# Raw q and k transposed together, and split into parts afterwards by GpSimd

## The chip, the cores and the metric

The kernel runs on one core of a Trainium2 chip. A core has five engines that run their own instruction streams and meet at semaphores: TensorE (PE; its weight loads are listed apart, as PEld), VectorE (DVE), ScalarE (ACT), GpSimd (POOL) and SyncE (SP), from whose queue this kernel issues all its DMA transfers. The metric is device time in microseconds (us).

## What is computed

Attention with a bucket mask, and two feed-forward blocks behind it. For each of 2 x 8 heads (768 tokens, head dimension 64):

```python
q_bits = (einsum('bhsd,dk->bhsk', q, proj) > 0)      # proj: 64 x 6
k_bits = (einsum('bhsd,dk->bhsk', k, proj) > 0)
q_bucket, k_bucket = sum(q_bits * 2**arange(6)), sum(k_bits * 2**arange(6))
mask = q_bucket[..., :, None] == k_bucket[..., None, :]
scores = where(mask, q @ k.T / sqrt(64), -1e9)
attn = softmax(scores); o = attn @ v                 # [768, 64] per head
```

Then `h = (x @ w1) * (x @ w2)`, `x = h @ w3 @ w_out`, and four experts `relu(x @ w1[e]) @ w2[e]`, weighted and summed. All inputs and the output are float32.

## The kernel before

**Precision.** PE multiplies in the type fp32r. To keep float32 accuracy, every operand is split into a high part (`tensor_copy` into an fp32r tile) and a low part (the value minus its high part), and a product is the sum of high x high, high x low and low x high.

**Order of the work.** In the opening part (to about 66 us) `w3` is transposed and multiplied with `w_out`; the preparation of heads 0 and 1 is put between these matmuls (`first_prep(n)`, n from 0 to 13). Then comes attention, head by head: heads 0 and 1 unrolled, the next in a loop over pairs of heads, the last pair unrolled. Behind it come the gates (the two products with `moe_w1` and `moe_w2`), the product with w3 x w_out, and the experts. Each engine has an `attention(i, first, last)` in which the order of its work for one head, m = 2i + s, is written out by hand. "Stretch of a head" below means the time in which PE goes once through this order. For head m PE does:

score tiles 3 to 5 of head m, score tiles 0 to 2 of head m+1 (`scores`), six tiles of transposed exponentials (`transpose_exps`), the products with v (`multiply_pv`), and, spread over the stretch, the preparation of head m+2 (`prep`, `project_parts`) up to the first half of its one-hot codes; the second half comes at the start of the next stretch.

**Preparation of a head.** SP loads raw q and raw k (`load_qk`, 192 KB each, two heads ahead of their use). GpSimd splits each into high and low parts side by side, so that `q_parts` holds [q_hi | q_lo] and `k_parts` [k_lo | k_hi] for each of the six token tiles (`split_q`, `split_k`, lines 471 to 487). PE transposes the twelve tiles of 128 x 128 into one PSUM bank, `ps_prep`, three at a time: steps j = 0 to 3 of `prep` (L1373). ACT copies each three out (`prep_copy`, L720) into `q_cross` = [q_hi; q_lo] and `k_cross` = [k_lo; k_hi] (rows 0 to 63; rows 64 to 127). GpSimd stacks both high parts in `q_main` (`stack_highs`, L496). PE projects them (`project_parts`, L1390, and step j = 4, L1379), DVE turns the signs into `bits` (L996), PE multiplies these with the bucket codes in steps 5 and 6 (L1382), and DVE makes one-hot rows of them (`onehot`, L1000). SP moves the high part of k to rows 0 to 63 of `k_main` (`move_high`), and the one-hot rows into rows 64 to 127 of `q_main` and `k_main` (`move_onehots`), all from SBUF to SBUF (L328). A score tile is then q_main x k_main + q_cross x k_cross (L1410, L1412): the one-hot rows carry the mask.

**DVE and ACT in a stretch.** Per score tile DVE scales it and takes its extreme (`scale_scores`, L1006), ACT takes the exponential (`exp_tile`, L724). There is one score buffer (two PSUM banks), so `scores` waits until the tile before is scaled. Per tile of transposed exponentials ACT writes the high part (`pT_high`, L732) and DVE the low part (`pT_low`, L1024). ACT copies the lower half of a product with v (`o_lower`, L737, tile `o_low`), and DVE adds it to the upper half (`o_sum`, L1032). Once per head DVE adds 1e-9 to the six row sums (`guard_sums`, L1012: a tensor_scalar of 128 x 6 from SBUF to SBUF) and takes their reciprocals (L1018). The middle of DVE's order for a head reads:

```python
scale(1, 0); add_parts(-1, 1); guard_sums(m, s); pT_low(6*m + 3, 3)
scale(1, 1); reciprocals(m, ...); pT_low(6*m + 4, 4); scale(1, 2)
encode(2, 4); pT_low(6*m + 5, 5)
```

**GpSimd in a stretch.** `split_q`, `split_k` of head m+2, `split_v` of head m+1 (L506, L508), `stack_highs` of head m+2; in every second stretch `x_scale` (L517, two tensor_tensor on the output of the pair before), and from head 9 on `first_parts`, which prepares the gates' first operand (among it L558 and L560, a copy and a subtraction of 128 x 768). Behind attention GpSimd combines the first gate weights (L587 to L594) and splits them (L623, L625).

**SP in a stretch.** `move_onehots` (head m+1), `load_v`, `move_high` (head m+2), `load_qk` (head m+4), `spread_reciprocals` (row sums' reciprocals to DRAM, wait, and back, L319 and L323). These are in one queue, each with its waits.

Of the kernel before, what the change touches and what calls it, by code (L numbers as in the profile page):

```python
# [7 lines left out]
F32 = mybir.dt.float32  # L8
# [12 lines left out]
def build_program(nc, q, k, v, proj, moe_w1, moe_w2, moe_w3, moe_w_out, probs, moe2_w1, moe2_w2,  # L21
# [15 lines left out]
    GROUPS = 7  # L37
# [32 lines left out]
    with ExitStack() as ctx:  # L70
# [104 lines left out]
        raw_q = [place(f"raw_q{s}", [P, TILES, DH], F32, prep_at) for s in range(2)]  # L175
        raw_k = [place(f"raw_k{s}", [P, TILES, DH], F32, prep_at) for s in range(2)]
        q_parts = [place(f"q_parts{s}", [P, TILES, P], F32R, prep_at) for s in range(2)]
        k_parts = [place(f"k_parts{s}", [P, TILES, P], F32R, prep_at) for s in range(2)]
        proj_w = [place(f"proj_w{n}", [P, P], F32R, prep_at) for n in range(6)]
# [55 lines left out]
        v_loaded = [sem(f"v_loaded{n}") for n in range(2)]  # L235
        stacks_moved = [sem(f"stacks_moved{n}") for n in range(2)]
# [6 lines left out]
        gate_step, pool_held = sem("gate_step"), sem("pool_held")  # L243
# [3 lines left out]
        q_hi_done, k_hi_done, v_hi_done = sem("q_hi_done"), sem("k_hi_done"), sem("v_hi_done")  # L247
        q_split, k_split, v_split = sem("q_split"), sem("k_split"), sem("v_split")
        prep_mm, prep_copied, prep_coded = sem("prep_mm"), sem("prep_copied"), sem("prep_coded")
        prep_open, highs_stacked = sem("prep_open"), sem("highs_stacked")  # L250
# [31 lines left out]

        def up_step(e, h, j):
            return GATE_ALL + ROUND_STEPS * (ROUNDS * e + h) + j
# [13 lines left out]
        def _(sp):  # L298
# [27 lines left out]
            def move(s, *pairs):  # L326
                for dst, src in pairs:
                    sp.dma_start(dst.bitcast(F32), src.bitcast(F32)).then_inc(stacks_moved[s], 16)  # L328

            def move_high(m, s):  # L330

                sp.wait_ge(prep_copied, 4 * m + 4)
                move(s, (k_main[s][0:DH, :], k_cross[s][DH:P, :]))

            def move_onehots(m, s):

                sp.wait_ge(prep_coded, 3 * m + 3)
                move(s, (q_main[s][DH:P, :], onehot[0:DH, :]), (k_main[s][DH:P, :], onehot[DH:P, :]))
# [64 lines left out]
            def attention(i, first, last):  # L403

                for s in range(2):
                    if s or not first:
                        move_onehots(2 * i + s + 1, 1 - s)
                    load_v(i + 1, s, False)
                    move_high(2 * i + 2 + s, s)
                    if not last:  # L410
                        load_qk(i + 2, s, False)
                    spread_reciprocals(2 * i + s, i, s, first)

            for s in range(2):
                move_high(s, s)
                move_onehots(s, s)
# [11 lines left out]
            sp.wait_ge(q_split, HEADS)  # L428
# [37 lines left out]
        def _(pool):  # L466
# [4 lines left out]
            def split_q(m, i, s, first):  # L471

                if not first:
                    pool.wait_ge(prep_mm, GROUPS * (m - 2) + 4)
                pool.wait_ge(qk_loaded[s], 32 * (i + 1))
                held()
                nc.gpsimd.tensor_copy(q_parts[s][:, :, 0:DH], raw_q[s][:, :, :]).then_inc(q_hi_done, 1)
                pool.wait_ge(q_hi_done, m + 1)
                nc.gpsimd.tensor_tensor(q_parts[s][:, :, DH:P], raw_q[s][:, :, :],
                                        q_parts[s][:, :, 0:DH].bitcast(F32), ALU.subtract).then_inc(q_split, 1)  # L480

            def split_k(m, s):

                nc.gpsimd.tensor_copy(k_parts[s][:, :, DH:P], raw_k[s][:, :, :]).then_inc(k_hi_done, 1)
                pool.wait_ge(k_hi_done, m + 1)
                nc.gpsimd.tensor_tensor(k_parts[s][:, :, 0:DH], raw_k[s][:, :, :],
                                        k_parts[s][:, :, DH:P].bitcast(F32), ALU.subtract).then_inc(k_split, 1)

            def stack_highs(m, s, values):


                pool.wait_ge(v_split, values)
                for part, (rows, src) in enumerate(((slice(0, DH), q_cross), (slice(DH, P), k_cross))):
                    pool.wait_ge(prep_copied, 4 * m + 2 * part + 2)
                    held()
                    nc.gpsimd.tensor_copy(q_main[s][rows, :], src[s][rows, :].bitcast(F32)).then_inc(highs_stacked, 1)  # L496
                    pool.wait_ge(highs_stacked, 2 * m + part + 1)
                held()

# [20 lines left out]
            for n in range(6):  # L520
                nc.gpsimd.memset(proj_w[n][:, :].bitcast(F32), 0.0).then_inc(zeros_set, 1)
# [3 lines left out]
            for s in range(2):  # L525
                split_q(s, 0, s, True)
                split_k(s, s)
            split_v(0, 0, 0, True)
            for s in range(2):
                stack_highs(s, s, 1)  # L530
# [32 lines left out]
            def attention(i, first, last, parts=()):  # L563
                for s in range(2):
# [11 lines left out]
                    if not last:  # L576
                        stack_highs(m + 2, s, m + 2)
# [39 lines left out]

            pool.wait_ge(prep_mm, GROUPS * (HEADS - 1) + 4)
            pool.wait_ge(k_split, HEADS)
# [79 lines left out]
        def _(act):  # L699
# [15 lines left out]
            def prep_copy(m, s, j):  # L715

                act.wait_ge(prep_mm, GROUPS * m + j + 1)
                dst = (q_cross if j < 2 else k_cross)[s]
                half = slice((j % 2) * HALF, (j % 2 + 1) * HALF)
                nc.scalar.copy(dst[:, half], ps_prep[:, 0:HALF]).then_inc(prep_copied, 1)  # L720
# [24 lines left out]
            def attention(i, first, last):  # L745

                for s in range(2):
# [23 lines left out]
                    copy(2, 2)  # L771
# [4 lines left out]
                    copy(2, 3)  # L776
# [14 lines left out]
            def first_copy(n):  # L791
                if n % GROUPS < 4:
                    prep_copy(n // GROUPS, n // GROUPS, n % GROUPS)
# [176 lines left out]
        def _(dve):  # L970
# [20 lines left out]
            def prep_code(m, j):  # L991

                half = slice((j - 5) * HALF, (j - 4) * HALF)
                dve.wait_ge(prep_mm, GROUPS * m + j + 1)
                if j == 4:
# [46 lines left out]
            def attention(i, first, last):  # L1042

                for s in range(2):
# [14 lines left out]
                    encode(1, 5)  # L1059
                    scale(0, 3)  # L1060
                    add_parts(-1, 0)
                    encode(1, 6)
# [15 lines left out]
                    encode(2, 4)  # L1078
                    pT_low(6 * m + 5, 5)

            def constants():

                dve.wait_ge(const_loaded, 16 * (4 + B))
                dve.wait_ge(zeros_set, 7)
                nc.vector.tensor_copy(code[:, :, :], code_f[:, :, :]).then_inc(code_ready, 1)


                cols = [slice(c, c + BITS) for c in (0, KBIT, DH, DH + KBIT)]
                for n in range(4):
                    nc.vector.tensor_copy(proj_w[n + n // 2][:, cols[n]], proj_f[:, :]).then_inc(proj_hi_ready, 1)  # L1090
                dve.wait_ge(proj_hi_ready, 4)
                for n in range(4):
                    rows = slice(0, DH) if n % 2 == 0 else slice(DH, P)
                    nc.vector.tensor_tensor(proj_w[3 * (n // 2) + 2][rows, cols[n]], proj_f[rows, :],
                                            proj_w[n + n // 2][rows, cols[n]].bitcast(F32), ALU.subtract)\
                        .then_inc(proj_ready, 1)
# [10 lines left out]
            def first_code(n):  # L1107
                if n == GROUPS + 5:
                    dve.wait_ge(stacks_moved[0], 48)
                if n % GROUPS >= 4:  # L1110
                    prep_code(n // GROUPS, n % GROUPS)
# [209 lines left out]
        def _(pe):  # L1321
# [35 lines left out]
            def prep(m, s, j, first):  # L1357

# [3 lines left out]
                elif 1 <= j < 4:  # L1362
                    pe.wait_ge(prep_copied, 4 * m + j)
                elif j > 4:
                    pe.wait_ge(prep_coded, 3 * m + j - 4)
                if j == 0:
                    pe.wait_ge(q_split, m + 1)
                if j == 2:
                    pe.wait_ge(k_split, m + 1)
                if j < 4:  # L1370
                    parts = (q_parts if j < 2 else k_parts)[s]
                    for tt in range(HT):
                        last = nc.tensor.transpose(ps_prep[:, tt * P:(tt + 1) * P],  # L1373
                                                   parts[:, (j % 2) * HT + tt, :].bitcast(F32), ident[:, :])
                elif j == 4:

                    pe.wait_ge(highs_stacked, 2 * m + 2)
                    for h in range(2):
                        last = nc.tensor.matmul(ps_prep[:, 0:HALF], proj_w[3 * h + 2][:, :],  # L1379
                                                q_main[s][:, h * HALF:(h + 1) * HALF], start=False, stop=h == 1)  # L1380
                else:
                    last = nc.tensor.matmul(ps_prep[:, 0:HALF], code[:, j - 5, :], bits[:, :], start=True, stop=True)  # L1382
                last.then_inc(prep_mm, 1)

            def project_parts(m, s):

                pe.wait_ge(prep_copied, 4 * m + 4)
                for h in range(2):
                    for n, src in enumerate((q_cross, k_cross)):
                        nc.tensor.matmul(ps_prep[:, 0:HALF], proj_w[3 * h + n][:, :],  # L1390
# [318 lines left out]
```

## Time and profile before

| | |
|---|---|
| median of 3 runs | 992.93 us (992.86 to 993.02) |
| the profiled execution | 992.96 us |
| its span, first to last instruction | 991.2 us |
| PE busy | 984.3 us (99%) |
| DVE busy | 626.4 us (63%) |
| ACT busy | 464.3 us (47%) |
| GpSimd busy | 436.7 us (44%) |
| granted TensorE clock | 1.0 of full speed all through |
| attention, heads 0 to 15 | about 66 to 306 us |

Busy shares are averages over parts with different limits: DVE's 63% is 14.0 of 15.1 us in a head's stretch and far less in the experts. Rows below give times in us from the span's start; in a timeline a row is start, duration, engine, line, operation, tiles and shapes, and in square brackets the idle time of the engine ahead of it with what ended it.

### The profile page before, as it was taken

To read this page: it belongs to the slowest core of one execution; us is meant where nothing else is said; L and a number is where in the kernel's file an instruction comes from. 1 tells how busy PE (TensorE), PEld (TensorE's weight loads), DVE (VectorE), ACT (ScalarE), POOL (GpSimd) and SP (SyncE) were. 2 spreads that over 40 slices of the span, in tenths; PEclk is the share of its full clock that TensorE was granted. 3 is DMA by queue.
4 is the path that set the end of the run, shared out by engine and by line. 5 is a ranking of instruction groups with operands and counts; after the bars stand their busy time and mean duration, and the time that the engine had idled before them with its cause. 6 is when DMAs were issued, how large, how long until landed. Compare 5 with 4: busy or idle time off the path is not lost.

```text
span 991.2 us, 15991 instructions
## 1 busy us (share of the span) xinstructions
PE 984.3 (99%) x5494; PEld 917.4 (93%) x5494; DVE 626.4 (63%) x964; ACT 464.3 (47%) x853; POOL 436.7 (44%) x446
## 2 busy tenths in 40 slices
PE   9999999999999999999999999999999999999998
PEld 7889999999989999999998998989989899898997
DVE  6359999999997995598755352544535545355342
ACT  4248888888875543555542340422404224042230
POOL 4024445367797991694263160431604316043130
PEclk9999999999999999999999999999999999999999
DMA  6223333232233220101100111001110011010102
GB/s 245 88 65 89 90 103 87 80 107 86 70 84 93 64 64 22 43 22 43 44 22 22 55 31 43 22 22 50 37 36 29 21 45 40 31 32 21 43 22 105
DMA packets 57646, 57.44 MB, mean 58 GB/s; under 512 B 7552, under 2 KB 46592, under 8 KB 57600
## 3 DMA queue, kind: packets, MB, share of 16 engines
q1 hardware_dynamic: 57600, 56.85, 19.2%
q8 instruction: 26, 0.43, 0.2%
q14 instruction: 20, 0.16, 0.1%
HBM read 44.20 MB, written 3.19 MB: 48 GB/s over the span
## 4 chain that ended last, share of the span: by engine, by line
PE 98%; DVE 1%; ACT 0%; issue 0%
PE ps L291 24%; PE ps L292 24%; PE ps L293 24%; PE ps L1423 6%; PE ps L1410 3%; PE ps L1438 3%; PE ps L1412 3%; PE ps L1440 3%; PE ps L1373 2%; PE ps L1390 1%; PE ps L1332 1%; PE ps L1379 1%; PE ps L1325 1%; PE ps L1382 1%; DVE pT_lo L1024 0%; DVE expo L1006 0%
## 5 line engine op out<-in xcount | busy, mean ns | idle before, releaser
L636 POOL TENSOR_TENSOR v_sum<-kept,kept 128x384 f32<-128x384 f32 x48 | 51.8, 1080 | 287.3 <-ACT kept L822 287.3
L822 ACT COPY kept<-ps 128x384 f32<-128x384 f32 x144 | 67.7, 479 | 206.4 <-PE ps L293 205.4
L1300 DVE SCALAR_TENSOR_TENSOR acc<-ps,gate,acc 128x512 f32<-128x512 f32 x96 | 72.0, 750 | 139.5 <-PE ps L293 139.5
L293 PE MATMUL ps<-v_hi,hid_lo 128*128 128x512 f32 x384 | 149.6, 390 | 0.0
L292 PE MATMUL ps<-v_lo,hid_hi 128*128 128x512 f32 x384 | 149.5, 389 | 0.0
L291 PE MATMUL ps<-v_hi,hid_hi 128*128 128x512 f32 x384 | 149.4, 389 | 0.0
L1006 DVE TENSOR_SCALAR_CACHE_REDUCE expo<-ps 128x768 f32<-128x768 f32 x96 | 91.7, 956 | 14.2 <-PE ps L1412 10.6
L724 ACT ACTIVATE expo<-expo,neg_max 128x768 f32<-128x768 f32 x96 | 90.7, 945 | 5.9 <-DVE expo L1006 4.5
L1024 DVE TENSOR_TENSOR pT_lo<-ps,pT_hi 128x768 fp32r<-128x768 f32 x96 | 90.5, 947 | 1.6 <-ACT pT_hi L732 1.1
L1149 DVE TENSOR_TENSOR u_sum<-ps,kept 128x384 f32<-128x384 f32 x48 | 26.6, 554 | 100.5 <-PE ps L293 100.5
L732 ACT CAST pT_hi<-ps 128x768 fp32r<-128x768 f32 x96 | 76.9, 804 | 24.2 <-PE ps L1423 23.9
L293 PEld LDWEIGHTS ps<-v_hi,hid_lo 128*128 128x128 f32 x384 | 72.1, 188 | 14.9
L291 PEld LDWEIGHTS ps<-v_hi,hid_hi 128*128 128x128 f32 x384 | 72.1, 188 | 14.9
L292 PEld LDWEIGHTS ps<-v_lo,hid_hi 128*128 128x128 f32 x384 | 72.1, 188 | 14.8
L1287 DVE SCALAR_TENSOR_TENSOR hid_lo<-c,hid_hi 128x384 fp32r<-128x384 f32 x96 | 56.5, 601 | 36.5 <-ACT hid_hi L942 19.1
L1423 PE MATMUL ps<-ident,expo 128*128 128x128 f32 x576 | 75.7, 273 | 1.0 <-DVE pT_lo L1024 1.0
L291 PE MATMUL ps<-xc_hi,w_hi 128*128 128x384 f32 x224 | 75.8, 338 | 0.6 <-ACT kept L822 0.6
L292 PE MATMUL ps<-xc_lo,e_hi 128*128 128x384 f32 x224 | 75.7, 338 | 0.0
L293 PE MATMUL ps<-xc_hi,e_lo 128*128 128x384 f32 x224 | 75.7, 338 | 0.0
L293 PE MATMUL ps<-xc_hi,w_lo 128*128 128x384 f32 x224 | 75.7, 338 | 0.0
L292 PE MATMUL ps<-xc_lo,w_hi 128*128 128x384 f32 x224 | 75.7, 338 | 0.0
L291 PE MATMUL ps<-xc_hi,e_hi 128*128 128x384 f32 x224 | 75.7, 338 | 0.0
(164 smaller groups left out, 2529.6 us busy)
## 6 DMA issues: line engine op xcount, KB each, us to landing
w_raw<-in_moe_w SPq DMA_DIRECT2D x64, 128.0 KB, 2.4
e_raw<-in_moe_w SPq DMA_DIRECT2D x64, 128.0 KB, 2.4
v_raw<-in_moe_w SPq DMA_DIRECT2D x32, 256.0 KB, 3.1
w_raw<-in_moe_w SPq DMA_DIRECT2D x8, 512.0 KB, 3.7
raw_q<-in_q SPq DMA_DIRECT2D x16, 192.0 KB, 2.6
raw_k<-in_k SPq DMA_DIRECT2D x16, 192.0 KB, 2.6
raw_v<-in_v SPq DMA_DIRECT2D x16, 192.0 KB, 2.7
k_main<-k_cross SPq DMA_DIRECT2D x16, 192.0 KB, 2.7
```

Of the source, the lines that this page charges most:

```text
L291: nc.tensor.matmul(out_ps, lhs_hi, rhs_hi, start=start, stop=False, skip_group_check=onto)
L292: nc.tensor.matmul(out_ps, lhs_hi, rhs_lo, start=False, stop=False, skip_group_check=onto)
L293: return nc.tensor.matmul(out_ps, lhs_lo, rhs_hi, start=False, stop=stop, skip_group_check=onto)
L636: nc.gpsimd.tensor_tensor(v_sum[:, :], kept[s][1][:, :], kept[s][2][:, :], ALU.add).then_inc(v_done, 1)
L724: nc.scalar.activation(expo[slot][:, :], expo[slot][:, :], ACT.Exp, scale=-1.0, bias=neg_max[:, slot:slot + 1], accum_out=row_sum[s][:, t: ...
L732: nc.scalar.copy(dst, ps_pT[t % 2][:, :, 0:HALF].rearrange("p a (c n) -> p a c n", n=P))\
L822: nc.scalar.copy(kept[s][n][:, :], ps[4 * s + n][:, 0:HALF]).then_inc(kept_done, 1)
L1006: nc.vector.tensor_scalar(expo[slot][:, :].rearrange("p (a n) -> p a n", a=2), ps_score[:, :, 0:HALF], -SCALE, None, ALU.mult, ALU.min, ac ...
L1024: nc.vector.tensor_tensor(pT_lo[half][:, :, cols].rearrange("p (a c) n -> p a c n", a=2), ps_pT[t % 2][:, :, 0:HALF].rearrange("p a (c n) ...
L1287: nc.vector.scalar_tensor_tensor(hid_lo[:, tile, cols], src, 0.0, hid_hi[:, tile, cols].bitcast(F32), ALU.max, ALU.subtract).then_inc(hid_ ...
L1300: nc.vector.scalar_tensor_tensor(acc[:, t, :], ps[4 * ((h + t // 4) % 2) + t % 4], gate_f[:, bass.ds(t * E + e, 1)], acc[:, t, :], ALU.mul ...
L1423: last = nc.tensor.transpose(ps_pT[t % 2][:, kt // HT, (kt % HT) * P:(kt % HT + 1) * P], expo[slot][:, kt * P:(kt + 1) * P], ident[:, :])
```

## The change

Raw q and raw k of a head lie side by side in one tile, `raw_qk` ([128, 6 tiles, 2, 64], float32). PE transposes the six tiles of 128 x 128, three at a time, in steps 0 and 1; ACT copies each three into `qk_T`, of which rows 0 to 63 are q and rows 64 to 127 are k, still float32. When both halves are there, GpSimd copies the whole to `q_main` (high parts, [q_hi; k_hi]) and subtracts into `q_cross` (low parts, [q_lo; k_lo]): 128 x 768 each. The projection is rearranged to match, with as many matmuls as before: `project_highs` multiplies `q_main` with the high and low parts of `proj`, step 2 multiplies `q_cross` with the high ones. Steps 3 and 4 are the former 5 and 6. The parts are then brought to their rows by transfers: `move_k` (three: `k_main` and `k_cross` rows 0 to 63, `k_cross` rows 64 to 127) and `move_q` (one, `q_cross` rows 64 to 127, behind the projection and behind `move_k`'s landing), in place of `move_high`'s one. The loads of q and k write pieces of 64 floats, with a gap of 64 between them. PE's order in a stretch is the one before without the former steps 2 and 3; ACT's is without their copies.

```diff
             def load_qk(i, s, first):
                 if not first:
-                    sp.wait_ge(k_split, 2 * i + s - 1)
-                for raw, heads in ((raw_q, q_heads), (raw_k, k_heads)):
-                    sp.dma_start(raw[s][:, :, :].rearrange("p t d -> p (t d)"), heads[2 * i + s, :, :])\
+                    sp.wait_ge(prep_mm, GROUPS * (2 * i + s - 2) + 2)
+                for n, heads in enumerate((q_heads, k_heads)):
+                    sp.dma_start(raw_qk[s][:, :, n, :], heads[2 * i + s, :, :].rearrange("p (t d) -> p t d", d=DH))\
                         .then_inc(qk_loaded[s], 16)
...
-            def move_high(m, s):
-                sp.wait_ge(prep_copied, 4 * m + 4)
-                move(s, (k_main[s][0:DH, :], k_cross[s][DH:P, :]))
+            def move_k(m, s):
+                sp.wait_ge(qk_hi_done, m + 1)
+                move(parts_moved[s], (k_main[s][0:DH, :], q_main[s][DH:P, :]), (k_cross[s][0:DH, :], q_main[s][DH:P, :]))
+                sp.wait_ge(qk_split, m + 1)
+                move(parts_moved[s], (k_cross[s][DH:P, :], q_cross[s][DH:P, :]))
+
+            def move_q(m, i, s):
+                sp.wait_ge(parts_moved[s], 48 * (i + 1))
+                sp.sem_inc(sp_held, 1)
+                sp.wait_ge(prep_mm, GROUPS * m + 3)
+                move(stacks_moved[s], (q_cross[s][DH:P, :], q_main[s][0:DH, :]))
...
                     load_v(i + 1, s, False)
-                    move_high(2 * i + 2 + s, s)
+                    move_k(2 * i + 2 + s, s)
                     if not last:
                         load_qk(i + 2, s, False)
                     spread_reciprocals(2 * i + s, i, s, first)
+                    move_q(2 * i + 2 + s, i + 1, s)
...
+            def split_qk(m, s):
+                pool.wait_ge(prep_copied, 2 * m + 2)
                 held()
-                nc.gpsimd.tensor_copy(q_parts[s][:, :, 0:DH], raw_q[s][:, :, :]).then_inc(q_hi_done, 1)
...
+                nc.gpsimd.tensor_copy(q_main[s][:, :], qk_T[s][:, :]).then_inc(qk_hi_done, 1)
+                pool.wait_ge(qk_hi_done, m + 1)
+                held()
+                nc.gpsimd.tensor_tensor(q_cross[s][:, :], qk_T[s][:, :], q_main[s][:, :].bitcast(F32), ALU.subtract)\
+                    .then_inc(qk_split, 1)
...
                     if not last:
-                        split_q(m + 2, i + 1, s, False)
-                        split_k(m + 2, s)
+                        split_qk(m + 2, s)
...
-            def project_parts(m, s):
-                pe.wait_ge(prep_copied, 4 * m + 4)
+            def project_highs(m, s):
+                pe.wait_ge(prep_copied, 2 * m + 2)
+                pe.wait_ge(qk_hi_done, m + 1)
                 for h in range(2):
-                    for n, src in enumerate((q_cross, k_cross)):
...
+                    for n, w in enumerate((proj_hi, proj_lo)):
+                        nc.tensor.matmul(ps_prep[:, 0:HALF], w[h][:, :], q_main[s][:, h * HALF:(h + 1) * HALF],
+                                         start=h + n == 0, stop=False)
```

`held` is an increment of a semaphore that nobody waits for; it stands between two waits of an engine. In the opening part heads 0 and 1 keep their places in the order, with two of the seven places per head now empty, and GpSimd's first work is `split_v` of head 0.

## Rows read from the trace of the kernel before

**Rows 1.** The page: busy time of each engine.
```profile
PE 984.3 (99%) x5494; PEld 917.4 (93%) x5494; DVE 626.4 (63%) x964; ACT 464.3 (47%) x853; POOL 436.7 (44%) x446
```

**Rows 2.** Busy time by engine in one head's stretch of the steady loop.
```profile
186.40:201.50 15.10, 15.10 (x106) 14.69 (x105) 14.02 (x26) 13.01 (x26) 6.39 (x9) 1.00 0.33 91
```

**Rows 3.** The chain of waits: first three transpositions of two successive heads.
```profile
191.79 0.33 PE ps L1373 x3
...
206.86 0.33 PE ps L1373 x3
```

**Rows 4.** Timeline of DVE in that stretch: start, duration, work, idle before.
```profile
194.55 0.96 DVE L1006 TENSOR_SCALAR_CACHE_REDUCE expo<-ps 128x768 f32<-128x768 f32 x1
...
196.00 0.55 DVE L1032 TENSOR_TENSOR x_raw<-ps,o_low 64x384 f32 x1 [0.49 <-ACT o_low L737]
...
196.58 0.17 DVE L1012 TENSOR_SCALAR guarded<-row_sum 128x6 f32<-128x6 f32 x1
...
196.72 0.96 DVE L1024 TENSOR_TENSOR pT_lo<-ps,pT_hi 128x768 fp32r<-128x768 f32 x1
...
197.60 0.95 DVE L1006 TENSOR_SCALAR_CACHE_REDUCE expo<-ps 128x768 f32<-128x768 f32 x1
```

**Rows 5.** Timeline of PE and its weight loads in that stretch.
```profile
193.65 0.34 PE L1410 MATMUL ps<-k_main,q_main 128*128 128x384 f32 x1
...
198.65 0.42 PE L1410 MATMUL ps<-k_main,q_main 128*128 128x384 f32 x1
...
201.18 0.10 PEld L1382 LDWEIGHTS ps<-bits,code 128*128 128x128 bf16 x1 [0.16 <-DVE bits L996]
```

**Rows 6.** Timeline of ACT in that stretch.
```profile
193.50 0.48 ACT L720 CAST q_cross<-ps 128x384 fp32r<-128x384 f32 x1
...
194.87 0.49 ACT L720 CAST k_cross<-ps 128x384 fp32r<-128x384 f32 x1
...
195.38 0.48 ACT L737 COPY o_low<-ps 64x384 f32<-64x384 f32 x1
...
196.58 0.49 ACT L720 CAST k_cross<-ps 128x384 fp32r<-128x384 f32 x1
```

**Rows 7.** POOL: starts behind its waits (timeline), then groups by line and form.
```profile
197.22 0.83 POOL L496 CAST q_main<-k_cross 64x768 fp32r<-64x768 f32 x1 [0.64 <-ACT k_cross L720]
...
290.50 0.74 POOL L594 TENSOR_TENSOR w_raw<-w_raw 128x256 f32<-128x256 f32 x1 [0.18 <-POOL w_raw L591]
...
L560 POOL TENSOR_TENSOR xc_lo<-s_raw,xc_hi 128x768 fp32r<-128x768 f32 x4 | 7.4, 1850 | 0.3
```

**Rows 8.** Line L1012's durations (min/median/max), then timelines of DVE and POOL.
```profile
L1012 DVE TENSOR_SCALAR guarded<-row_sum x16: 153/172/705, 76.1 to 300.0; 128x6 f32<-128x6 f32 x16
...
285.88 2.35 POOL L517 TENSOR_TENSOR x_raw<-x_raw,rec_rows 128x384 f32<-128x384 f32 x2
...
286.40 0.70 DVE L1012 TENSOR_SCALAR guarded<-row_sum 128x6 f32<-128x6 f32 x1
...
298.55 1.83 POOL L625 TENSOR_TENSOR w_lo<-w_raw,w_hi 128x768 fp32r<-128x768 f32 x1
...
299.99 0.42 DVE L1012 TENSOR_SCALAR guarded<-row_sum 128x6 f32<-128x6 f32 x1
```

**Rows 9.** Timelines of POOL and PE where attention hands over to the gates.
```profile
273.54 0.83 POOL L558 CAST xc_hi<-s_raw 128x768 fp32r<-128x768 f32 x1 [0.17 <-POOL q_main L496]
...
297.80 0.42 PE L291 MATMUL ps<-xc_hi,w_hi 128*128 128x384 f32 x1
```

**Rows 10.** The page's DMA issues (median us to landing), SP's timeline, then tile k_main.
```profile
e_raw<-in_moe_w SPq DMA_DIRECT2D x64, 128.0 KB, 2.4
...
190.36 0.59 SPq L328 DMA_DIRECT2D k_main<-onehot  x1
...
201.19 0.54 SPq L323 DMA_DIRECT2D rec_rows<-sum_reciprocals  x1
...
DMA to landing us min/median/max: 2.5/2.9/4.5
```

More of the change, by code:

```diff
@@ L173, in build_program @@
         assert rec_at[0] <= cursor[0]
[L175 to L179, printed above, removed]
+        raw_qk = [place(f"raw_qk{s}", [P, TILES, 2, DH], F32, prep_at) for s in range(2)]
+        qk_T = [place(f"qk_T{s}", [P, S], F32, prep_at) for s in range(2)]
+        proj_hi = [place(f"proj_hi{h}", [P, P], F32R, prep_at) for h in range(2)]
+        proj_lo = [place(f"proj_lo{h}", [P, P], F32R, prep_at) for h in range(2)]
         onehot = place("onehot", [P, S], F32R, prep_at)
@@ L235, in build_program @@
         v_loaded = [sem(f"v_loaded{n}") for n in range(2)]
+        parts_moved = [sem(f"parts_moved{n}") for n in range(2)]
         stacks_moved = [sem(f"stacks_moved{n}") for n in range(2)]
@@ L412, in attention @@
                     spread_reciprocals(2 * i + s, i, s, first)
+                    move_q(2 * i + 2 + s, i + 1, s)
             for s in range(2):
-                move_high(s, s)
+                move_k(s, s)
+                move_q(s, 0, s)
                 move_onehots(s, s)
@@ L519, in _ @@
             nc.gpsimd.memset(ident[:, :], 0.0).then_inc(zeros_set, 1)
-            for n in range(6):
-                nc.gpsimd.memset(proj_w[n][:, :].bitcast(F32), 0.0).then_inc(zeros_set, 1)
+            for part in (*proj_hi, *proj_lo):
+                nc.gpsimd.memset(part[:, :].bitcast(F32), 0.0).then_inc(zeros_set, 1)
             pool.wait_ge(zeros_set, 1)
@@ L524, in _ @@
                                     pattern=[[-1, P]], channel_multiplier=1).then_inc(ident_ready, 1)
[L525 to L527 removed]
             split_v(0, 0, 0, True)
             for s in range(2):
[L530 removed]
+                split_qk(s, s)
             def first_parts(step):
@@ L717, in prep_copy @@
                 act.wait_ge(prep_mm, GROUPS * m + j + 1)
-                dst = (q_cross if j < 2 else k_cross)[s]
-                half = slice((j % 2) * HALF, (j % 2 + 1) * HALF)
-                nc.scalar.copy(dst[:, half], ps_prep[:, 0:HALF]).then_inc(prep_copied, 1)
+                nc.scalar.copy(qk_T[s][:, j * HALF:(j + 1) * HALF], ps_prep[:, 0:HALF]).then_inc(prep_copied, 1)
             def exp_tile(g, slot, s, t):
@@ L1366, in prep @@
                 if j == 0:
[L1367 to L1371, printed above, removed]
+                    pe.wait_ge(qk_loaded[s], 32 * (i + 1))
+                if j < 2:
                     for tt in range(HT):
[L1373 to L1377, printed above, removed]
+                        last = nc.tensor.transpose(ps_prep[:, tt * P:(tt + 1) * P], raw_qk[s][:, j * HT + tt, :, :].rearrange("p n d -> p (n d)"),
+                                                   ident[:, :])
+                elif j == 2:
+                    pe.wait_ge(qk_split, m + 1)
@@ L1378, in prep @@
                     for h in range(2):
-                        last = nc.tensor.matmul(ps_prep[:, 0:HALF], proj_w[3 * h + 2][:, :],
-                                                q_main[s][:, h * HALF:(h + 1) * HALF], start=False, stop=h == 1)
+                        last = nc.tensor.matmul(ps_prep[:, 0:HALF], proj_hi[h][:, :],
+                                                q_cross[s][:, h * HALF:(h + 1) * HALF], start=False, stop=h == 1)
                 else:
-                    last = nc.tensor.matmul(ps_prep[:, 0:HALF], code[:, j - 5, :], bits[:, :], start=True, stop=True)
+                    last = nc.tensor.matmul(ps_prep[:, 0:HALF], code[:, j - 3, :], bits[:, :], start=True, stop=True)
```

113 lines of the change are left out of this document (43 added, 70 removed).

## The prediction

> **What bounds the kernel now.** I read the page first: PE is busy for 984.3 us, 99% of the span [rows 1], so PE work that goes should be time that goes. Then I went to the stretches that the change touches, since a share over the span hides other limits there. While one head is attended, the stretch holds 15.10 us of PE work and, beside it, 14.02 us of DVE work [rows 2]. One head follows the other after 206.86 - 191.79 = 15.07 us [rows 3]. PE is the bound, with DVE only 1.1 us behind it, so the question is how the two engines are coupled.
>
> The timelines answer that for the second half of a head, in which all of the change's transpositions lie. DVE scales a score tile (L1006, 194.55), idles 0.49 us until ACT has copied `o_low`, adds (196.00), guards the row sums (L1012, 196.58), forms `pT_lo` (196.72) and scales the next tile (197.60 to 198.55) [rows 4]. `scores` waits for that scaling, since there is one score buffer, and PE's next score matmul starts at 198.65 [rows 5]: no slack. At 201.18 PE waits again, 0.16 us, for DVE's `bits` [rows 5]. So in this half of the head PE runs in DVE's step, and PE work taken out there is worth only what DVE gets earlier.
>
> **The change, part by part.** All times are of the stretch above; it stands for the 14 heads' stretches in which a head two ahead is prepared.
>
> PE: six of twelve transpositions per head go. Three take 0.33 us of the chain [rows 3], one 0.11. In the loop, 84 of them leave PE 0.66 us per head free. In the opening part, heads 0 and 1 are prepared between matmuls of the weight product, with nothing near them that PE waits for: 12 x 0.11 = 1.3 us gained there. The four matmuls of `project_highs` and the two of step 2 cost what `project_parts` and step 4 did.
>
> ACT: the two `k_cross` copies go. The first (194.87 to 195.36) stood right ahead of the `o_low` copy (195.38) [rows 6], which moves up by 0.49 us. That is DVE's idle time: its addition could then start when the scaling ends, at 195.54 in place of 196.00, and the guard at 196.12. PE meets the next scores 0.66 us earlier, so it isn't late for DVE's scaling. With nothing else in the way a head would take 0.46 us less.
>
> GpSimd: per head four splits and two stacking copies go; one copy 128x768 and one subtraction 128x768 come. The row of the copy says 0.83 us [rows 9], that of the same subtraction 1.85 us [rows 7]. Both wait for the second transposed half, whose copy ends at 193.50 + 0.48 = 193.98 [rows 6]. GpSimd started 0.15 us behind the ACT copy that ended at 196.58 + 0.49 = 197.07 [rows 6], at 197.22, and 0.18 us behind its own result when a wait and a `held` lie between [rows 7]. So: copy 194.13 to 194.96, subtraction 195.14 to 196.99. PE wants the copy in `project_highs`, which stands behind scores that wait for the scaling's end at 195.54: hidden by 0.6 us at least. It wants the subtraction behind the scores of 198.65: hidden by 1.7 us. Were that cover gone, each us late would be a us per head.
>
> But the guard would now start at 196.12, inside that subtraction. L1012 takes 0.15 to 0.25 us in fourteen heads, and 0.70 and 0.42 in two [rows 8]. In those two GpSimd was in a tensor_tensor: two of them from 285.88, the first over at about 285.88 + 2.35/2 = 287.06, the guard at 287.10; one over at 298.55 + 1.83 = 300.38, the guard at 300.41 [rows 8]. The guard ends 0.03 us behind the GpSimd instruction that it met, wherever in it it came. The `pT_lo` and PSUM-reading instructions show nothing of the sort: L1024 keeps to 0.96 us [rows 4]. So the new guard should last from 196.12 to 197.02, and `pT_lo` starts at about 196.94, against 196.72 before. DVE comes out 0.22 us later, not 0.46 earlier; with up to 0.06 us of slack at the score wait I take 0.21. Scores, scaling, `bits` and the code matmul behind them follow, each coupled as above, and the next head starts 0.21 us later: 14 x 0.21 = +2.9 us. Bounds per head: -0.46 (the guard isn't held) and +0.30 (subtraction late by a tenth).
>
> The Trainium skill, Advanced Engine Details and Errata, section VectorE Performance Modes, says that an instruction of VectorE that uses two ports (source and destination in SBUF) and GpSimd's instructions block each other, as the second port is shared. The guard is the one such instruction in the loop, and the two long guards agree; by a reading in which only GpSimd gives way, the sum would be that of the rival "the guard is free".
>
> GpSimd at the end of attention: its first copy of the parts that follow head 15's preparation starts at 273.54, and from there to PE's first gate matmul at 297.80 GpSimd is busy without a gap; PE gets there just as its operand is ready [rows 9]. The new order ends the preparation later: counted from 186.5, the subtraction is over at 10.5, and `split_v` (a copy and a subtraction of half the width, so a bit over half their 2.86 us, an estimate) and the starts behind it take until 12.25. In head 13's stretch, which begins five periods later at 261.85, that copy came at 11.7. It comes 0.55 later, of which PE itself loses 0.2: +0.35 us once.
>
> SP: three more transfers per head, each of the form of `k_main<-k_cross`. `move_k` ends its waits with the subtraction at 196.99, where `move_high` waited until 197.07; queued behind it are `load_qk` and the reciprocals, which nobody needs soon. `move_q` waits last, behind the reciprocals' round trip, whose last transfer was issued at 201.19 for 0.54 us [rows 10] and now comes 0.2 later: `move_q` has issued by about 202.4, one period earlier 187.3. `move_onehots` is next behind it, its two transfers issued about half a us apart, the second at 190.36 [rows 10]: 2.5 us to spare. The second lands 2.9 us later, 193.26 [rows 10], against scores that run at 193.65 [rows 5] with weights loaded 0.17 earlier: about 0.2 us of slack, unchanged, price 0. `load_qk` now writes 256 B pieces in place of 1,536 B ones. Loads in 512 B pieces land in 2.4 us (128 KB), moves in 3,072 B pieces in 2.9 (192 KB) [rows 10]: small pieces don't show in the landing. I take 0, since the loads have a whole head of time; the upper bound is a rival.
>
> Sum: -1.3 + 2.9 + 0.35 = +2.0 us. The profiled execution took 992.96 us (span 991.2 and 1.8 around it), the runs' median 992.93, so nothing is to be corrected: 994.9 us.
>
> **The rivals.**
>
> The guard is free. For it: two rows are few, and neither has a GpSimd subtraction from this very tile. Against it: both ends agree to 0.03 us. Then each of 14 heads gains 0.46 us, the opening 1.3, and the hand-over to the gates costs 1.0 (GpSimd 0.55 late, PE 0.46 early): 992.96 - 6.4 - 1.3 + 1.0 = 986.3.
>
> All PE time counts. For it: 99% [rows 1]. Against it: DVE's coupling at 198.65 and 201.18 [rows 5]. It gives 96 x 0.11 = 10.5 us, 982.5.
>
> The loads in small pieces hold up the queue. Raw loads stand ahead of the reciprocals' round trip, `move_q` and the onehots. Up to 2.7 us (2.5 + 0.2) of longer loads per head are free; from there PE waits at the first score of each head. At 4 us it would lose 1.3 us, and 14 heads 18 us, with the forecast's other terms 1013. Against it: the small pieces above.
>
> The Trainium skill, DMA: Bandwidth & Descriptors, section Specifications, gives 512 B as the least piece for full rate, with a read-modify-write below it. That speaks for this rival; no transfer of 256 B pieces is in this trace.
>
> **How the numbers follow.** The guard held: 0.65, own range 992.4 to 996.8 (low: 0.05 per head, 1.3 off, no hand-over; high: 0.30 per head, 1.0 off, hand-over 0.6). The guard free: 0.18. All PE time: 0.05. The queue held up: 0.12. About 0.2% (2.0 us) is what a measurement of this kernel can tell from no change: below 991.0 is faster, above 994.9 slower. The forecast lies on that edge, so its 0.65 goes to 0.31 slower, 0.32 same, 0.02 faster. Faster 0.25, same 0.32, slower 0.43. The range takes in the free guard, 985.2 to 998.0, and leaves out all PE time and most of the held queue.
>
> **What would show it.** L1012 at 0.8 to 0.95 us in the heads' stretches, ending with GpSimd's new subtraction; heads 15.2 to 15.35 us apart; no wait of PE for GpSimd in the loop; the opening 1.3 us shorter. Wrong would be: L1012 near 0.17 and heads 14.6 us apart; a wait of PE for an onehot transfer; a subtraction well off 1.85 us.

## The result, and the profile of the changed kernel

The changed kernel takes 996.42 us (median of 7 runs, 995.64 to 997.81), the kernel before 993.02 (7 runs, 992.58 to 994.25): ratio 1.0036 [1.0025 to 1.0048], slower by 0.36%. The forecast was 994.9 us, its range 985.2 to 998.0. The profiled execution took 995.64 us, its span is 993.8 against 991.2, +2.6.

The page of the changed kernel, first busy time by engine, then the DMA queue (packets, MB, share of 16 engines):
```profile
PE 978.9 (99%) x5398; PEld 905.3 (91%) x5398; DVE 633.6 (64%) x964; ACT 451.8 (45%) x821; POOL 403.5 (41%) x380
...
q1 hardware_dynamic: 81920, 66.29, 24.2%
```
Against [rows 1] PE lost 96 instructions and 5.4 us of busy time, ACT 12.5 us, GpSimd 33.2 us. DVE has the instructions that it had, 964, and 7.2 us more busy time. No work was given to it, so some instruction of it got longer. Which one shows in the groups for lines L997 (the guard, L1012 before), L1003 (the reciprocal) and L494 (GpSimd's new subtraction), in ns min/median/max:
```profile
L997 DVE TENSOR_SCALAR guarded<-row_sum x16: 424/947/1382, 74.4 to 302.4; 128x6 f32<-128x6 f32 x16
...
L1003 DVE RECIPROCAL row_rec<-guarded x16: 179/180/183, 77.0 to 304.0; 128x6 f32<-128x6 f32 x16
...
L494 POOL TENSOR_TENSOR q_cross<-qk_T,q_main x16: 1832/1842/1852, 23.4 to 272.7; 128x768 fp32r<-128x768 f32 x16
```
The same 128 x 6 instruction took a median of 172 ns before [rows 8] and takes 947 now.

Timeline of the stretch that answers to the one of [rows 3] to [rows 7], all engines, in order of time. First transpositions stand at 192.69 and 207.97: 15.28 us apart.
```profile
192.69 0.49 PE L1353 MATMUL ps<-ident,raw_qk 128*128 128x128 f32 x3
...
194.57 0.48 ACT L707 COPY qk_T<-ps 128x384 f32<-128x384 f32 x1
195.22 0.83 POOL L491 CAST q_main<-qk_T 128x768 fp32r<-128x768 f32 x1 [10.89 <-ACT qk_T L707]
...
195.62 0.96 DVE L991 TENSOR_SCALAR_CACHE_REDUCE expo<-ps 128x768 f32<-128x768 f32 x1
...
196.23 1.84 POOL L494 TENSOR_TENSOR q_cross<-qk_T,q_main 128x768 fp32r<-128x768 f32 x1 [0.18 <-POOL q_main L491]
...
196.62 0.55 DVE L1017 TENSOR_TENSOR x_raw<-ps,o_low 64x384 f32 x1
...
197.21 0.89 DVE L997 TENSOR_SCALAR guarded<-row_sum 128x6 f32<-128x6 f32 x1
198.01 0.94 DVE L1009 TENSOR_TENSOR pT_lo<-ps,pT_hi 128x768 fp32r<-128x768 f32 x1
...
199.10 0.85 PE L1405 MATMUL ps<-ident,expo 128*128 128x128 f32 x6 [0.44 <-DVE pT_lo L1009]
...
207.97 0.49 PE L1353 MATMUL ps<-ident,raw_qk 128*128 128x128 f32 x3
```
The reader is to see three things. The idle time ahead of DVE's addition (0.49 us in [rows 4]) is gone: it follows the scaling at once. The guard then starts 0.98 us into the subtraction, which ends at 196.23 + 1.84 = 198.07, and ends itself at 198.10. And PE, which stood still for nobody there before, waits 0.44 us for the `pT_lo` behind the guard. The table of the stretch (busy time of PE, PEld, DVE, ACT, POOL) and the waits of the whole span say the same, 7.1 us in 13 places:
```profile
192.69:207.97 15.28, 14.84 (x100) 14.03 (x98) 14.53 (x25) 12.19 (x24) 6.47 (x6) 1.00 0.53 132
...
PE ps L1405 <- DVE pT_lo L1009: 7.1, 13, 1.0
```
PE is busy for 0.23 us less in this window than the 15.07 of before, and the window is 0.21 us longer.

**Where the time went, on the trace.** The first transposition of head 2 moved from 71.29 to 69.97 (-1.32, the opening). The 13 periods from there to the last prepared head add up to 199.17 us against 195.66 (+3.51). From there to the first gate product, 300.26 against 297.80 [rows 9], another 0.27 was lost, and the rest, between 0.1 and 0.2, behind it: +2.6 together.

### The profile page after: what moved, and what is told of

It is laid out like the page before. It is cut to its first block, busy times and chain, and to the rows that moved or that the text cites. A ratio compares the mean times of both kernels' runs of the same rounds, so it can differ in the third digit from the quotient of the medians.

```text
span 993.8 us, 15662 instructions
## 1 busy us (share of the span) xinstructions
PE 978.9 (99%) x5398; PEld 905.3 (91%) x5398; DVE 633.6 (64%) x964; ACT 451.8 (45%) x821; POOL 403.5 (41%) x380
## 4 chain that ended last, share of the span: by engine, by line
PE 63%; POOL 1%; issue 0%; ACT 0%; DVE 0%; POOLq 0%; ACTq 0%
PE ps L295 21%; PE ps L296 21%; PE ps L297 21%; POOL w_raw L578 0%; POOL c L646 0%; POOL w_raw L582 0%; POOL a L631 0%; ACT w_hi L730 0%; POOL c L631 0%; POOL v_sum L625 0%; ACT kept L807 0%; POOL w_raw L585 0%; DVE acc L1283 0%; POOLq L484 0%; POOL w_raw L579 0%
## 5 line engine op out<-in xcount | busy, mean ns | idle before, releaser
L991 DVE TENSOR_SCALAR_CACHE_REDUCE expo<-ps 128x768 f32<-128x768 f32 x96 | 91.7, 955 | 14.6 <-PE ps L1394 11.1
L1009 DVE TENSOR_TENSOR pT_lo<-ps,pT_hi 128x768 fp32r<-128x768 f32 x96 | 90.3, 945 | 1.2 <-ACT pT_hi L719 1.2
L491 POOL CAST q_main<-qk_T 128x768 fp32r<-128x768 f32 x16 | 13.2, 824 | 162.8 <-ACT qk_T L707 162.8
L1405 PEld LDWEIGHTS ps<-ident,expo 128*128 128x128 f32 x576 | 65.7, 140 | 14.3 <-ACT expo L711 11.7
```

Source lines behind the costliest of these rows:

```text
L991: nc.vector.tensor_scalar(expo[slot][:, :].rearrange("p (a n) -> p a n", a=2), ps_score[:, :, 0:HALF], -SCALE, None, ALU.mult, ALU.min, ac ...
L1009: nc.vector.tensor_tensor(pT_lo[half][:, :, cols].rearrange("p (a c) n -> p a c n", a=2), ps_pT[t % 2][:, :, 0:HALF].rearrange("p a (c n) ...
L1405: last = nc.tensor.transpose(ps_pT[t % 2][:, kt // HT, (kt % HT) * P:(kt % HT + 1) * P], expo[slot][:, kt * P:(kt + 1) * P], ident[:, :])
```

## Experiments

A period is the time from one head's first transposition to the next's. Ratios are to the kernel before, measured in the same session. All edits are to the changed kernel unless said otherwise.

**1. No guard.** The addition of 1e-9 is left out and the reciprocal reads the row sums themselves.
```diff
-                nc.vector.tensor_scalar(guarded[:, :], row_sum[s][:, :], EPS, None, ALU.add).then_inc(sums_guarded, 1)
+                dve.sem_inc(sums_guarded, 1)
...
-                nc.vector.reciprocal(row_rec[:, :], guarded[:, :]).then_inc(rec_done, 1)
+                nc.vector.reciprocal(row_rec[:, :], row_sum[s][:, :]).then_inc(rec_done, 1)
```


> The changed kernel with the guard of the row sums left out: the reciprocals are taken of the row sums as they are (what is left out is the addition of 1e-9). If DVE's wait for GpSimd's subtraction is what turned the change into a loss: DVE gets its 0.46 us back and the guard's own 0.1, heads go from 15.28 to 14.5 us apart, and the whole to 986.5 us (14 heads x 0.76 and the odd starts of the subtraction off, the hand-over to the gates 0.8 on). If the loss comes from the transfers, the small load pieces or GpSimd's own lateness: heads stay near 15.3 us apart and the whole at 995 to 997.

988.72 us, ratio 0.9958 [0.9941 to 0.9975]: from slower to faster by one instruction of six columns. Ten of the 13 periods are 14.46 to 14.63 us, three 14.92 to 15.04. GpSimd's subtraction is as long as ever, and `pT_lo` (L1009) starts inside it:
```profile
189.89 0.96 DVE L991 TENSOR_SCALAR_CACHE_REDUCE expo<-ps 128x768 f32<-128x768 f32 x1
190.42 1.84 POOL L494 TENSOR_TENSOR q_cross<-qk_T,q_main 128x768 fp32r<-128x768 f32 x1 [0.18 <-POOL q_main L491]
...
191.53 0.96 DVE L1009 TENSOR_TENSOR pT_lo<-ps,pT_hi 128x768 fp32r<-128x768 f32 x1
...
291.52 0.41 PE L295 MATMUL ps<-xc_hi,w_hi 128*128 128x384 f32 x1 [1.24 <-issue]
```
`pT_lo` starts 1.64 us behind the scaling, where it was 2.39 in the changed kernel. The last row is the first gate product: with the heads shorter, PE gets there 1.24 us before its operand. In each of the three long periods PE waits for a transfer of one-hot rows (0.20, 0.23 and 0.34 us), of which experiment 5 shows more. The expectation was missed by 2.2 us: the periods are 14.6 and not 14.5, three of them are longer, and behind the first gate product this execution takes 2.1 us more than the changed kernel's, in waits among the gates (below). PE's wait ahead of that product was priced at 0.8.

**2. The kernel before without its guard**, as the control: the same edit to it.

> The kernel before with the guard left out (what is left out is the addition of 1e-9), the control for e1. There the guard takes 0.17 us and the tile that follows it waits for ACT until 0.14 us behind the guard's start, so nothing should be gained per head: 991.5 to 993 us, with about 0.7 us to be had only in the last two heads, where it met GpSimd. If leaving the guard out is worth as much here as in e1, the wait for GpSimd is not the change's own cost.

993.14 us, ratio 0.9999 [0.9990 to 1.0009]; periods 15.07. The guard's own 0.17 us is worth nothing. So experiment 1 is not the price of an instruction but of its wait. First gate product:
```profile
295.61 2.38 POOL L625 TENSOR_TENSOR w_lo<-w_raw,w_hi 128x1024 fp32r<-128x1024 f32 x1
...
298.09 0.42 PE L291 MATMUL ps<-xc_hi,w_hi 128*128 128x384 f32 x1 [0.74 <-issue]
```
In the last heads, where the guard took 0.70 and 0.42 [rows 8], PE came free sooner, and then waited 0.74 us. The profile names no releaser for that wait, but the product starts 0.10 us behind the end of GpSimd's first low part of the gate weights (295.61 + 2.38 = 297.99), and so it does in all twelve profiles. The hand-over to the gates goes by GpSimd.

**3. The subtraction in two halves** of 128 x 384.
```diff
-                nc.gpsimd.tensor_tensor(q_cross[s][:, :], qk_T[s][:, :], q_main[s][:, :].bitcast(F32), ALU.subtract)\
+                nc.gpsimd.tensor_tensor(q_cross[s][:, t0], qk_T[s][:, t0], q_main[s][:, t0].bitcast(F32), ALU.subtract)\
+                    .then_inc(half_split, 1)
+                nc.gpsimd.tensor_tensor(q_cross[s][:, t1], qk_T[s][:, t1], q_main[s][:, t1].bitcast(F32), ALU.subtract)\
```


> The changed kernel with GpSimd's subtraction 128x768 made as two of 128x384. If the guard waits for the end of the one GpSimd instruction that it meets: the first half should be over at about the time at which the guard starts, so L997 falls from 0.95 to 0.1 to 0.3 us, heads come to 14.6 to 14.7 us apart, the whole to about 988 us. If the guard has to wait until GpSimd is idle: no change or slower by the extra instruction, 996 to 998.

992.81 us (10 runs), ratio 0.9994 [0.9984 to 1.0004]: no change that could be measured, and 5 us more than expected. The periods alternate between about 14.63 and 15.40. Two neighbouring stretches, GpSimd's halves (L495, L497) and the guard (L1000):
```profile
178.52 1.01 POOL L495 TENSOR_TENSOR q_cross<-qk_T,q_main 128x384 fp32r<-128x384 f32 x1 [0.19 <-POOL q_main L492]
179.38 0.18 DVE L1000 TENSOR_SCALAR guarded<-row_sum 128x6 f32<-128x6 f32 x1
179.49 1.02 POOL L497 TENSOR_TENSOR q_cross<-qk_T,q_main 128x384 fp32r<-128x384 f32 x1
...
193.14 1.00 POOL L495 TENSOR_TENSOR q_cross<-qk_T,q_main 128x384 fp32r<-128x384 f32 x1 [0.18 <-POOL q_main L492]
194.11 1.01 POOL L497 TENSOR_TENSOR q_cross<-qk_T,q_main 128x384 fp32r<-128x384 f32 x1
194.12 1.03 DVE L1000 TENSOR_SCALAR guarded<-row_sum 128x6 f32<-128x6 f32 x1
```
A guard that is there 0.11 us before the second half starts slips in at the seam and costs 0.18; one that comes 0.01 behind its start waits it out, 194.11 + 1.01 = 195.12 against 195.15. The length of the wait is the rest of the one instruction met. My expectation had the guard meet the first half always; where in GpSimd's work it falls was known only to a tenth, and that tenth decided. The tenth is in the kernel before too: the guard starts 0.58 us behind the start of DVE's addition in one head and 0.47 in the next, in turn, in every profile with a guard on DVE. The 0.58 are the heads in which that addition writes rows 64 to 127, and the guard then starts behind the addition's end instead of 0.08 us ahead of it; why is not shown.

**4. The guard as a tensor_tensor**, which adds a tile that holds 1e-9: the same work on two operands in SBUF.
```diff
-                nc.vector.tensor_scalar(guarded[:, :], row_sum[s][:, :], EPS, None, ALU.add).then_inc(sums_guarded, 1)
+                nc.vector.tensor_tensor(guarded[:, :], row_sum[s][:, :], eps_t[:, :], ALU.add).then_inc(sums_guarded, 1)
```


> The changed kernel with the guard as a tensor_tensor with a tile of 1e-9 (two SBUF inputs) in place of a tensor_scalar. If only the two-port form of a one-input instruction is held: the guard takes about 0.2 us and the whole comes to 987. If anything that reads through DVE's second SBUF port is held, two inputs too: no change, 995 to 997, guard near 0.95 us.

996.48 us, ratio 1.0042 [1.0026 to 1.0059]. It is held just as long:
```profile
L999 DVE TENSOR_TENSOR guarded<-row_sum,eps_t x16: 429/942/1359, 74.2 to 302.7; 128x6 f32<-128x6 f32 x16
```

**5. The guard on ACT.** The whole computation stands; ACT adds 1e-9, behind `pT_high` of tile 4.
```diff
+            def guard_sums(m, s):
+                if not isinstance(m, int) or m:
+                    act.wait_ge(rec_done, m)
+                act.wait_ge(exp_done, 6 * m + TILES)
+                nc.scalar.activation(guarded[:, :], row_sum[s][:, :], ACT.Copy, bias=EPS).then_inc(sums_guarded, 1)
...
                     pT_high(6 * m + 4, 4)
+                    guard_sums(m, s)
```


> The changed kernel with the whole computation kept and the guard moved to ACT, behind the fifth tile of transposed exponentials (pT_high 4), where ACT has idle time. If DVE's wait for GpSimd is the cost: as e1, about 987 us; ACT's 0.2 us per head are hidden. If ACT has become too tight: 988 to 991.

989.90 us, ratio 0.9971 [0.9959 to 0.9984]. The guard takes 216 to 242 ns on ACT. Most of the other periods are 14.6, but six of 13 are 14.86 to 15.49. What PE waits for in them, in this kernel's waits (us in total, times, longest):
```profile
PE ps L1398 <- DMA k_main<-onehot: 2.5, 6, 0.7
...
PEld ps L1398 <- DMA k_main<-onehot: 1.3, 2, 0.9
```
The one-hot rows come too late in all six. (The two rows count one of these waits twice, and one of PEld's, 0.40 us in the last heads, is in the kernel before too, with 0.38.) So the rival of the held-up queue shows once the heads are quicker. At 15.28 us it hardly does: the changed kernel's profile has no such wait in the 13 periods, the second profile of it (experiment 10) one of 0.39 us that lengthens no period, and experiment 4's one of 0.58 us, in a period of 15.70.

**6. The guard on ACT, and `move_q` issued earlier**: between the store of the reciprocals and the wait for it, where the queue stood idle.
```diff
                 sp.dma_start(sum_rec_tiles[m, :, :], row_rec[:, :]).then_inc(rec_stored, 16)
+                if between is not None:
+                    between()
                 sp.wait_ge(rec_stored, 16 * (m + 1))
...
-                    spread_reciprocals(2 * i + s, i, s, first)
-                    move_q(2 * i + 2 + s, i + 1, s)
+                    spread_reciprocals(2 * i + s, i, s, first, lambda: move_q(2 * i + 2 + s, i + 1, s))
```


> e5 with one more edit on SP's queue: move_q is issued between the reciprocals' store and the wait for it, in place of behind their read-back. In e5 PE waited 3.8 us in eight heads for an onehot transfer. If those land late because move_q's transfer and the read-back are issued right ahead of them: the waits fall under 1 us, all heads come to 14.6 us apart, the whole to 986 to 987 us. If they are late for DMA traffic in general: as e5, 990.

987.12 us, ratio 0.9944 [0.9929 to 0.9959]. Behind the first, all periods are 14.61 to 14.68: no long one is left. PE still waits 1.20 us at the first gate product.

**7. The same, with GpSimd's preparation of the gates a step earlier.**
```diff
-            attention(DK + 2, False, False, ((3,), (4, 5)))
-            attention(PAIRS - 1, False, True, (6, 7))
+            attention(DK + 2, False, False, ((3, 4), (5, 6)))
+            attention(PAIRS - 1, False, True, (7,))
```


> e8 with GpSimd's first_parts moved up: step 4 from head 13's stretch to head 12's, steps 5 and 6 in head 13's, only step 7 in head 14's. In e1 and e5 PE waited 1.2 us at the first gate product for GpSimd's split weights. If GpSimd's unbroken work there is what PE meets: the wait goes and the whole is 1.0 to 1.2 us below e8, about 985.5. If the weights' loads end last: as e8.

986.00 us (5 runs, 985.39 to 988.59), ratio 0.9941 [0.9927 to 0.9954]. First gate product:
```profile
290.51 0.42 PE L295 MATMUL ps<-xc_hi,w_hi 128*128 128x384 f32 x1 [0.24 <-issue]
```
It starts 1.44 us earlier than in experiment 6 (0.34 of that stands already in its opening), and the span is 1.4 shorter (984.1 against 985.5), though the intervals of the two ratios overlap. This version computes all that the reference does and is faster than both kernels: 0.6% less than the one before, and by the two ratios about 1% less than the changed one.

**8. The changed kernel with `move_q` earlier and nothing else.**

> The changed kernel with only SP's order changed as in e8. If the guard's wait sets the pace of the heads, the transfers do not: 995.5 to 997, as the changed kernel, perhaps with fewer slow runs. If late onehot transfers made the part of the loss that the profile of the fastest run does not show: 995 and a spread under 1 us.

996.84 us, ratio 1.0040 [1.0024 to 1.0055]: nothing gained. While the guard is held, the order of the queue isn't what sets the pace of the heads.

**9. The kernel before, with only its loads of q and k in 256 B pieces.**
```diff
-                for raw, heads in ((raw_q, q_heads), (raw_k, k_heads)):
-                    sp.dma_start(raw[s][:, :, :].rearrange("p t d -> p (t d)"), heads[2 * i + s, :, :])\
+                for n, heads in enumerate((q_heads, k_heads)):
+                    sp.dma_start(raw_qk[s][:, :, n, :], heads[2 * i + s, :, :].rearrange("p (t d) -> p t d", d=DH))\
```


> The kernel before, with only the loads of raw q and k written in pieces of 256 B into one tile, as in the changed kernel; GpSimd reads them with a gap. If small pieces cost time: above 993.5, with the onehot transfers landing late. If they are hidden: 992.5 to 993.5, landing of the loads 3.0 to 3.5 us in place of 2.6.

994.02 us (10 runs), ratio 1.0009 [0.9999 to 1.0019]; periods 15.07, and in them no wait of PE for a transfer. GpSimd's splits read the tile with the same gap, in the time that they took before (0.50 and 1.02 us). The loads land later, at a median of 3.3 us:
```profile
DMA to landing us min/median/max: 2.9/3.3/5.6
```
The same loads took 2.6 in the kernel before. At most 1.9 us of the change's cost can be this; the interval holds no change only nearly at its edge, and no stretch of the trace shows a cost.

**10. The changed kernel once more**, for a second profile.

> The changed kernel once more, for a second profile: its runs lie between 995.6 and 997.8 us, wider than before's, and the one profile is of the fastest. If the spread comes from GpSimd's late subtractions in the loop (0.55 and 0.28 us behind the copy in place of 0.18), a slower run shows more of them or longer ones; if from the transfers, PE's waits for them.

995.47 us, span 993.7, and the same order of long and short periods (15.67, 15.37 and 15.35 the three long ones). So the long periods aren't chance.

## Why the prediction was right, and where its sizes were off

Forecast 994.9, measured 996.42: inside the range and inside the likeliest case's own, 992.4 to 996.8, though 1.5 us too low. On the trace +2.6 us against the +2.0 forecast is in part luck: the heads were priced 0.8 us too low and the hand-over 0.3 too high.

**The coupling of the two engines: right, almost to the hundredth.** Counted from the start of the scaling in the stretch shown, in us:

| | forecast | measured |
|---|---|---|
| subtraction starts | 0.59 | 0.61 |
| guard starts | 1.57 | 1.59 |
| subtraction over | 2.44 | 2.45 |
| guard over | 2.47 | 2.48 |
| `pT_lo` starts | 2.39 | 2.39 |
| heads apart | 15.28 | 15.28 |

`pT_lo` stood at 2.17 before [rows 4], so the 0.22 per head is there. That the guard's wait is the cause was read from two rows of sixteen [rows 8] and is now shown: without the guard, or with it on another engine, the period is 14.61, the 0.46 us less that the prediction gave for "the guard is free"; the control without a guard in the kernel before gains nothing. The Trainium skill, Advanced Engine Details and Errata, section VectorE Performance Modes, gives the rule (a two-port instruction of VectorE and GpSimd's block each other); the traces agree, with a median of 0.17 us in the kernel before and up to 1.38 inside the subtraction. One sentence of the prediction was wrong: the guard is not "the one such instruction in the loop". The reciprocal too has its source and destination in SBUF, and it isn't held (last section). The kernel before showed that already, and the sum doesn't hang on it.

**The sum over the heads: right in kind, mis-sized.** "14 x 0.21 = +2.9" came out as 3.51 in 13 periods and most of another 0.27. Ten periods are 15.26 to 15.31. The rest is in two things that one stretch of the steady loop couldn't show. The first period was 14.86 before, not 15.07, and is 15.26 like the others now: 0.2 more. And three periods are 15.64, 15.38 and 15.36: 1.17 above 15.07 together, 0.54 more than three times 0.21. There the subtraction starts 0.55, 0.28 and 0.27 us behind the copy, not 0.18. These are the second heads of the three iterations of GpSimd's loop over pairs of heads (line 600), in every profile of the changed kernel and its variants but that of experiment 3, whose first half starts 0.2 us behind the copy throughout; what holds the start back isn't shown. In the longest:
```profile
118.30 0.82 POOL L491 CAST q_main<-qk_T 128x768 fp32r<-128x768 f32 x1 [8.57 <-ACT qk_T L707]
119.67 1.85 POOL L494 TENSOR_TENSOR q_cross<-qk_T,q_main 128x768 fp32r<-128x768 f32 x1 [0.55 <-POOL q_main L491]
120.17 1.38 DVE L997 TENSOR_SCALAR guarded<-row_sum 128x6 f32<-128x6 f32 x1
```
The guard ends with the subtraction again, 121.55 against 121.52, so what GpSimd loses there DVE and PE lose too. A "subtraction late by a tenth" was my upper bound per head, and 0.37 was met.

**The opening: right.** -1.32 measured, -1.3 forecast, and -1.41 in the second profile. It isn't a firm gain: in experiments 3, 5, 6 and 7, whose opening is the changed kernel's, head 2 starts 0.5 to 0.9 us later than in it, and PE waits there for a second load of `w_raw`, 0.35 to 0.98 us at about 19.5 us.

**The hand-over: too high.** +0.35 forecast. From the last preparation to the first gate product 0.27 was lost, and 0.21 of it is that stretch's own head, so 0.1 or less is left. GpSimd's first copy moved by 2.45 us and the product by 2.46, as the step has it: the product goes by GpSimd there (experiment 2). What was mis-sized is `split_v`: the forecast had it and the starts behind it take 1.75 us from the subtraction's end (10.5 to 12.25), an estimate. They took 1.48, from 272.67 + 1.84 = 274.51 to 275.99.
```profile
272.67 1.84 POOL L494 TENSOR_TENSOR q_cross<-qk_T,q_main 128x768 fp32r<-128x768 f32 x1 [0.18 <-POOL q_main L491]
...
275.99 0.82 POOL L552 CAST xc_hi<-s_raw 128x768 fp32r<-128x768 f32 x1
...
300.26 0.42 PE L295 MATMUL ps<-xc_hi,w_hi 128*128 128x384 f32 x1
```

**SP and the transfers at nothing: right for this kernel, as far as experiments 8 and 9 can tell.** The first gained nothing, and its interval leaves about 1.2 us at most for the queue's order; the second leaves at most 1.9 us for the pieces. `move_q` came later than forecast: its issue was over at 204.20, 1.7 us ahead of the one-hot rows' first transfer (205.92), not 2.5. The step "about 0.2 us of slack, unchanged" holds only while the heads are 15.28 apart: at 14.6 the one-hot rows came up to 0.9 us late (experiment 5), and moving `move_q` forward mended it (experiment 6). So the rival "the guard is free" would not have given 986.3 by itself; it gave 988.7 and 989.9, and 987.1 and 986.0 only with the queue and the gates' preparation mended.

**Between the profiled execution and the median.** By the trace the change costs 2.6 us, by the medians 3.4. The runs of the changed kernel spread over 2.2 us. The profiled execution of experiment 8 shows where such a difference can lie. It took 997.28 us with a span of 995.5, reached the first gate product 0.16 us earlier than the changed kernel's, and lost 1.5 us more in the gates, in waits for ACT's `kept`; its wait, one of the late places, and then the changed kernel's wait:
```profile
PE ps L295 <- ACT kept L808: 2.2, 3, 1.0
...
349.70 0.41 PE L295 MATMUL ps<-xc_hi,w_hi 128*128 128x384 f32 x1 [1.01 <-ACT kept L808]
```
```profile
PE ps L295 <- ACT kept L807: 0.7, 1, 0.7
```
Experiment 1's execution shows 2.5 us there. Ahead of these waits GpSimd's sum of 128 x 384 (L631, in experiment 8 L632) took 1.79 us in place of 1.13, beside DVE at an instruction between SBUF tiles. The place and the price are on the trace; that this is the same holding in the other direction is argued, not shown, and that the slower runs without a profile lose their time there stays open.

## What to carry to other kernels

Before work is moved onto GpSimd, look up which VectorE instructions between SBUF tiles will run beside it: a tensor_scalar or a tensor_tensor was held here to the end of the GpSimd instruction that it met, a reciprocal wasn't. So a 0.17 us instruction on the critical engine's path can cost most of a 1.84 us one, and the row of its duration (minimum against maximum over its calls) tells it before the change is made. Moving that small instruction to a third engine mended it here; cutting the large one in two did so in about every second head only. And when a stall is taken out, ask again who was late by less: here a DMA queue, worth 2.8 us by the medians (experiment 6 against 5), and the next part's preparation, worth about 1 (7 against 6, within the noise of the medians).

## What was unexpected about the hardware

- The reciprocal of the same 128 x 6 tile, SBUF to SBUF, isn't held: 179 to 183 ns in all 16 calls of the changed kernel. In the stretch of head 8 it runs inside GpSimd's pair of tensor_tensors:
```profile
199.55 2.40 POOL L514 TENSOR_TENSOR x_raw<-x_raw,rec_rows 128x384 f32<-128x384 f32 x2
199.75 0.18 DVE L1003 RECIPROCAL row_rec<-guarded 128x6 f32<-128x6 f32 x1
```
- By the same sign a GpSimd copy holds the guard too. In the kernel before, four of the fourteen short guards met the end of GpSimd's copy of 64 x 768; they took 0.21 to 0.25 us and ended 0.03 us behind it. The others took 0.15 to 0.17.
- A tensor_tensor with two SBUF inputs is held as the tensor_scalar is (experiment 4: median 942 ns against 947). The Trainium skill, SBUF — State Buffer, section SBUF: two separate sides, names both kinds, and that the loser waits for the whole instruction; the runs agree with both.
- Cutting the GpSimd instruction in two opens a seam, but DVE gets through it only when it is there first (experiment 3: 0.18 us when 0.11 early, 1.03 when 0.01 late).
